# Row maxima of the attention scores taken in two parts instead of one

## What is computed

```python
def _attn_ref(q, k, v):
    q_pool = q.reshape(B, H, S // factor, factor, D).mean(axis=3)
    scores = scale * np.matmul(q_pool, k.transpose(0, 1, 3, 2))
    scores = scores - np.max(scores, axis=-1, keepdims=True)
    attn = np.exp(scores)
    attn = attn / (np.sum(attn, axis=-1, keepdims=True) + 1e-09)
    return np.matmul(attn, v)
...
x = attn_out.transpose(0, 2, 1, 3).reshape(B * S, H * D)
h = x @ w_in
g = np.maximum(h, 0.0) + alpha * np.minimum(h, 0.0)
return g @ w_out
```

## Time and profile before

| what | us |
|---|---|
| median of 3 runs | 893.23 (893.14 to 893.24) |
| profiled execution | 892.93 |
| its span, first to last instruction | 891.2 |
| TensorE busy in it | 859.3 |
| VectorE busy | 514.0 |
| ScalarE busy | 422.1 |

### The profile page before, as it was taken

One profiled execution on the slowest core, in us unless ns is written; L12 is line 12 of the kernel. 1 busy time (PEld: TensorE's weight loads), 2 busy tenths in 40 slices (PEclk: granted clock), 3 DMA queues, 4 the chain that ended last, 5 costly groups with the idle time before them and its releaser, 6 DMA issues. The chain is left out here.

```text
span 891.2 us, 19945 instructions
## 1 busy us (share of the span) xinstructions
PE 859.3 (96%) x6577; PEld 613.0 (69%) x6577; DVE 514.0 (58%) x791; ACT 422.1 (47%) x936; POOL 205.2 (23%) x170
## 2 busy tenths in 40 slices
PE   6899999999999999999999999999999999999996
PEld 3455555555555555555557999998999998999985
DVE  4676777677777777767674344345444445344342
ACT  2666666666666666666663222224222224222222
POOL 3101010110101010110402322323233233322320
PEclk9999999999999999999999999999999999999999
DMA  8626543464435543464122122124222223322211
GB/s 194 147 65 153 130 115 96 114 152 98 124 97 137 134 110 100 111 152 109 51 85 70 59 60 70 60 61 128 64 67 59 62 68 100 90 60 70 59 35 71
DMA packets 42638, 84.37 MB, mean 95 GB/s; under 512 B 7536, under 2 KB 15728, under 8 KB 42608
## 3 DMA queue, kind: packets, MB, share of 16 engines
q1 hardware_dynamic: 40208, 79.28, 34.6%
q10 hardware_dynamic: 2400, 4.72, 1.6%
HBM read 79.18 MB, written 4.79 MB: 94 GB/s over the span
## 5 line engine op out<-in xcount | busy, mean ns | idle before, releaser
L743 PE MATMUL slot_ps<-ff 128*128 128x384 f32 x1152 | 218.0, 337 | 1.4 <-PEq L740 1.4
L743 PEld LDWEIGHTS slot_ps<-ff 128*128 128x128 f32 x1152 | 204.4, 188 | 11.1 <-issue 3.2
L529 DVE TENSOR_REDUCE neg_max<-s_ps 128x1 f32<-128x1152 f32 x144 | 194.7, 1352 | 19.9 <-DVEq L528 19.1
L759 PE MATMUL s_ps<-ff 128*128 128x512 f32 x720 | 182.4, 394 | 2.6 <-PEq L756 2.6
L657 PE MATMUL s_ps<-k_f,q_f 64*128 64x512 f32 (+1 forms) x640 | 164.3, 632 | 1.0 <-PEq L709 0.9
L435 ACT ACTIVATE e_sb<-s_ps,neg_max 128x1024 f32<-128x1024 f32 x144 | 159.8, 1110 | 0.0
L690 PE MATMUL pv_ps<-pt,v_f 128*64 128x256 f32 (+1 forms) x1152 | 155.1, 412 | 0.2 <-PEq L709 0.2
L759 PEld LDWEIGHTS s_ps<-ff 128*128 128x128 f32 x720 | 133.4, 188 | 27.1 <-issue 4.1
L690 PEld LDWEIGHTS pv_ps<-pt,v_f 128*64 128x64 f32 x1152 | 76.7, 136 | 95.8 <-issue 52.6
L581 DVE TENSOR_SCALAR e_sb<-slot_ps,alpha_sb 128x384 f32<-128x384 f32 x96 | 59.3, 617 | 115.1 <-DVEq L579 115.1
L353 POOL TENSOR_TENSOR q_raw<-q_raw 128x576 f32<-128x576 f32 x30 | 42.2, 1406 | 343.8 <-POOLq L352 343.8
(11 more groups left out here) (42 smaller groups left out, 511.5 us busy)
## 6 DMA issues: line engine op xcount, KB each, us to landing
k_f<-in_k SPq DMA_DIRECT2D x64, 288.0 KB, 4.3
q_raw<-in_q SPq DMA_DIRECT2D x62, 288.0 KB, 4.2
wi_raw<-in_w_in SPq DMA_DIRECT2D x48, 256.0 KB, 2.6
wo_raw<-in_w_out SPq DMA_DIRECT2D x48, 256.0 KB, 2.6
v_f<-in_v SPq DMA_DIRECT2D x32, 288.0 KB, 3.8
out<-pt ACTq DMA_DIRECT2D x6, 768.0 KB, 4.8
inv_bc<-sums SPq DMA_DIRECT2D x32, 80.0 KB, 3.7
k_end<-in_k SPq DMA_DIRECT2D x64, 32.0 KB, 3.9
```

Of the source, the lines that this page charges most:

```text
L529: nc.vector.tensor_reduce(out=neg_max[:, b:b + 1], in_=s_ps[:, S_AT[b]:S_AT[b] + NKEY], op=ALU.max, axis=AX_X, negate=True).then_inc(max_r ...
L743: ins = nc.tensor.matmul(slot_ps[h][:, 0:TOK], w[i][:, d * P:(d + 1) * P], x[h][:, d * TOK:(d + 1) * TOK], start=(d == 0 and w is wi_hi an ...
L759: ins = nc.tensor.matmul(y_ps[h][t], g[h][:, t * P:(t + 1) * P], w[i], start=(first == 0 and j == 0), stop=(last == 1 and j == 2))
```

## The change

`row_max` stays for the first two tiles only. For all others the maximum is formed in parts. `big_max(s + 2)` reduces the 1024 columns of the large piece into `neg_big`. In even steps it is placed ahead of the wait for bank 2 and the ninth copy. Behind that copy, `small_max` reduces the small pieces of both tiles s+2 and s+3, two runs of 128 columns in bank 2, by one instruction into two columns of `neg_small`; `both_max` waits for the reductions and joins the two parts with a minimum (the maxima are negated) of one column. In odd steps there are `big_max` and `both_max` alone, since the small piece's maximum is there. The semaphore `even_cut_done`, its wait on VectorE and its increment on ScalarE go, since an odd step's reduction no longer touches bank 2.

```diff
             def exponential_cut(s, done=None):
...
-                                     accum_out=row_sum[:, 0, SUM_AT[t]:SUM_AT[t] + 1]).then_inc(done, 1)
+                if done is not None:
+                    ins.then_inc(done, 1)
...
-                    exponential_cut(s + 1, even_cut_done)
+                    exponential_cut(s + 1)
...
+            def big_max(s):
+                b = s % 2
+                dve.wait_ge(s_ready, 2).then_inc(s_ready, -2)
+                nc.vector.tensor_reduce(out=neg_big[:, b:b + 1],
+                                        in_=s_ps[:, S_AT[b] + BIG_AT[b]:S_AT[b] + BIG_AT[b] + 2 * BANK],
+                                        op=ALU.max, axis=AX_X, negate=True).then_inc(max_self, 1)
+
+            def small_max():
+                cols = s_ps[:, 2 * BANK:3 * BANK].rearrange("p (i c) -> p i c", c=P)[:, 0:4:3, :]
+                nc.vector.tensor_reduce(out=neg_small[:, :], in_=cols, op=ALU.max, axis=AX_X,
+                                        negate=True).then_inc(max_self, 1)
+
+            def both_max(s, parts):
+                b = s % 2
+                dve.wait_ge(max_self, parts).then_inc(max_self, -parts)
+                nc.vector.tensor_tensor(neg_max[:, b:b + 1], neg_big[:, b:b + 1], neg_small[:, b:b + 1],
+                                        ALU.min).then_inc(max_ready, 1)
...
+                if left > 1 and s % 2 == 0:
+                    big_max(s + 2)
                 if s % 2 == 0:
                     dve.wait_ge(bank2_ready, 1).then_inc(bank2_ready, -1)
                     nc.vector.tensor_copy(ninth_columns(ninth_tiles(s)),
                                           ninth_blocks(ninth_tiles(s))).then_inc(ninth_free, 1)
                 if left > 1:
-                    if s % 2 == 1:
-                        dve.wait_ge(even_cut_done, 1).then_inc(even_cut_done, -1)
-                    row_max(s + 2)
+                    if s % 2 == 0:
+                        small_max()
+                        both_max(s + 2, 2)
+                    else:
+                        big_max(s + 2)
+                        both_max(s + 2, 1)
```

More of the change, by code:

```diff
@@ L84, in build @@
         neg_max = sb("neg_max", [P, 2])
+        neg_big = sb("neg_big", [P, 2])
+        neg_small = sb("neg_small", [P, 2])
         table = sb("table", [P, 1])
@@ L153, in build @@
         s_ready = sem("s_ready")
+        max_self = sem("max_self")
         max_ready = sem("max_ready")
         exp_cut_done = sem("exp_cut_done")
-        even_cut_done = sem("even_cut_done")
         exp_done = sem("exp_done")
@@ L423, in _, with exponential_cut @@
         def _(act):
-            def exponential_cut(s, done):
+            def exponential_cut(s, done=None):
                 t, b, e = s % TILES, s % 2, s % 3 * NKEY
@@ L427, in exponential_cut @@
                 act.wait_ge(max_ready, 1).then_inc(max_ready, -1)
-                nc.scalar.activation(e_sb[:, e + END[b][0]:e + END[b][0] + P], s_ps[:, at:at + P],
-                                     ACT.Exp, bias=neg_max[:, b:b + 1],
-                                     accum_out=row_sum[:, 0, SUM_AT[t]:SUM_AT[t] + 1]).then_inc(done, 1)
+                ins = nc.scalar.activation(e_sb[:, e + END[b][0]:e + END[b][0] + P], s_ps[:, at:at + P],
+                                           ACT.Exp, bias=neg_max[:, b:b + 1],
+                                           accum_out=row_sum[:, 0, SUM_AT[t]:SUM_AT[t] + 1])
+                if done is not None:
+                    ins.then_inc(done, 1)
             def exponential(s):
```

## The result

| kernel | median us (runs) | ratio to before, 95% interval |
|---|---|---|
| before | 893.13 (20) | |
| changed | 894.96 (20), 894.05 to 895.78 | 1.0021 (1.0014 to 1.0028) |

The changed kernel is 1.8 us slower: a loss of 0.2%, and outside the range 887.3 to 894.0. Its runs spread over 1.7 us, those of before over 0.65. Its profiled execution took 894.15 (span 892.4), 0.8 under its median.

The account below looks back on a forecast made before the run. TensorE, busy for 96% of the span, was taken as the bound, so only its waits could shrink: 0.9 + 0.2 + 0.6 + 0.7 = 2.4 us off the profiled 892.93 gives 890.5, median 890.8; range 887.3 to 894.0.

Parts of the forecast that it names:

- the price of the join: VectorE's minimum of both parts: 0.15 waiting plus 0.15 work, 0.30 us behind the reduction; bounds 0.15 and 0.50.
- a join over 0.40: Sign to look for in the profile after: such a join would make the forecast wrong towards slower.
- the walk: Start times followed through one attention cycle of 18 steps (two head pairs), with the new order and prices.
- Step 2: Cycle's third step: ninth-block transposes start at 196.20 rather than 195.76, 0.44 us lost, made up two steps later.
- step 6: Ninth-block transposes behind step 5's inversion: TensorE still waits about 0.9 us, starting at 208.20 against 208.32.
- The cycle: 18 attention steps of two head pairs: gains 0.03 us in steps 0 to 7, 0.08 and 0.09 at two later steps.
- The opening: First attention steps, 2 to 6, without products to hide waits: earlier maxima give 0.9 us, once.
- B: Rival, larger gain: no 0.15 gap ahead of a join, some 3 us more come through, 887.8 us; chance 0.15.
- C: Rival, no change: 0.24 idle ahead of the odd maximum is VectorE's restart behind the slot copy, 893.0 us; chance 0.25.
- D: Rival, slower: VectorE becomes the bound of steps 0 to 6, joins cost 0.50, 896.5 us; chance 0.15.
- step 10: In each cycle, the odd maximum behind step 9's inversion comes 0.08 us sooner: 8 x 0.08 = 0.6 us.
- steps 0 and 14: Even steps with scaling and inversion ahead of the ninth copy: the large piece makes the even maximum 0.5 us later.

Follow-up runs that it names:

- one-input kernel: The changed kernel with the join done as a reduction over two columns of one tile instead of a two-input operation: 890.64 us, ratio 0.9972.
- the old form with the two-input join: The changed kernel with one whole reduction and the old wait again in pairs of steps whose even step inverts: 895.27 us, ratio 1.0031.
- the pair of idle operations: The kernel before with an unused VectorE operation behind each row maximum but the first two, with two inputs or one: 894.5 and 892.75 us.

## Why the prediction was wrong, point by point

**The step that failed is the price of the join**, "0.15 of work", "0.15" from below and "0.50" from above. It was taken from the inversion's sum as the nearest row in kind. That sum also has two inputs in SBUF, but in the trace of before it met GpSimd only once, for the last 0.05 us of a subtraction (446.67), and took 0.152 to 0.156 in all 32 places, so its rows could not show that price. In the one-input kernel it met one for longer and took 0.398: the row was nearest in kind, down to the price that it hid. In the changed kernel the join costs 0.159 in 112 places and up to 2.25 in 30, and this is worth 894.96 - 890.64 = 4.3 us. The upper bound of 0.50 came from a restart that turned out not to exist, and the mean of the joins lies well under it: 0.27, or 0.42 with the gap. The prediction's own sign, a join over 0.40, appeared in 24 places. The mean was not the point; the walk looked at three engines and not at GpSimd, which was busy for 23% of the span and off the path.

The trace of before had the clue, outside attention. GpSimd's own subtractions in the network, by source line (shortest, median, longest), and the longest of them in the timeline with VectorE beside it:

```profile
L394 POOL TENSOR_TENSOR ff<-wo_raw,ff x48: 1271/1294/2363, 476.2 to 870.5; 128x512 fp32r<-128x512 f32 x48
```

```profile
607.92 1.76 DVE L622 TENSOR_TENSOR ff<-x_f,ff 128x1536 fp32r<-128x1536 f32 x1 [0.82 <-DVEq L621]
...
608.47 2.36 POOL L394 TENSOR_TENSOR ff<-wo_raw,ff 128x512 fp32r<-128x512 f32 x1 [3.98 <-POOLq L393]
```

VectorE ends at 609.68, and GpSimd's 2.36 end 1.15 later, a little less than its usual length of 1.29: there it was GpSimd that waited for a two-input instruction of VectorE. All four such instructions of VectorE in that trace find a subtraction of GpSimd, which takes 2.35 or 2.36. A longest of 2.36 beside a median of 1.29 is what should have led me there.

The Trainium skill, page "SBUF — State Buffer", section "Who interferes with whom", says that a VectorE instruction with two SBUF inputs contends with a GpSimd instruction that reads SBUF, since its second input comes through the shared read interface, that the order of issue decides who blocks, and that `tensor_reduce` never contends on trn2. The traces agree: joins that end 0.02 behind GpSimd's addition, the reverse at 608.47, and 0.155 to 0.157 for the reducing join. By that page's rule the two-input join was the wrong choice, and the prediction did not weigh it.

**What was right.** All from the kernel with the one-input join, unless said:
- The prices of the pieces, and 0.15 ahead of each join (21.7 us before 142 joins in that kernel).
- Step 2 loses 0.44: measured 0.43 in each cycle but the first (0.53). Step 4 makes it up, step 6 waits 0.84 (about 0.9 was said), and each start came within 0.05 of the walk. The ninth transposes of step 2 show no wait in brackets, though; the wait stands ahead of the big scores before them (0.28).
- The cycle: forecast 0.20 (0.03 + 0.08 + 0.09), measured 0.18 to 0.22 in each of five, and 0.46 in the first, which stays open. The opening: 0.9 forecast, 0.78 measured.
- The sum: 890.8 forecast, 890.64 measured. That it fits within 0.2 is in part luck. At its last instruction TensorE is 2.26 ahead of before: 0.78 from the opening and 1.48 from the next six cycles, less 0.21 by which it starts later and 0.19 from 418 us to the end of attention, and 0.4 more from the network (1.87 ahead at 600 us, 2.23 at 700), which the forecast had at nothing.
- In the changed kernel itself only the opening's gain came through, 0.77 at 70 us, although three joins had been long by then.

**The rivals.** B (no gap ahead of a join) is out: the gap is in all 142 places. C (a restart behind the slot copy) is out: after the change the odd large piece starts where the copy ends, at 193.20 behind 192.59 + 0.69, with no idle time.

```profile
192.59 0.69 DVE L587 COPY pt<-slot_ps 128x512 f32<-128x512 f32 x1
...
193.20 1.22 DVE L540 TENSOR_REDUCE neg_big<-s_ps 128x1 f32<-128x1024 f32 x1
```

D (VectorE as the bound) named the side on which it ended, and put the deciding point 0.1 above the join's 0.30. The mean excess, 16.0 / 142 = 0.11, lies at just that point. But its mechanism, a join of 0.50 everywhere, is not what happened: one in five was hit, by up to 2.1 us, and what it costs depends on whether TensorE needs that tile at that time. With the same order and a join of 0.155 the time is 890.64, so VectorE is not the bound that D meant. D's own terms, 890.8 + 5.6 + 0.6 for step 10, come to 897.0 and not to 896.5.

**What was left on the table.** The prediction priced the reordering at step 2 as a loss of 0.44 that is made up two steps later. It is made up only because waits there shrink anyway (0.54 from step 2 to step 4, with or without the loss): with the loss taken out, all of it comes through, 3.1 us. That was not a wrong number, but an order that the walk had already named as late ("that is steps 0 and 14") and that the experiments show to be worth undoing.

## What to carry to other kernels

Before a small VectorE operation with two SBUF inputs goes on a critical chain, look at what GpSimd does beside it, however idle that engine is, and at the longest and not only the mean duration of like rows; a reduction over two columns of one tile, or a per-partition scalar as second operand, cost the same or 0.06 more and was never held up. Splitting a reduction pays where the engine otherwise idles for the second part's input (even steps without an inversion ahead), and here hardly anywhere else: the best kernel, 885.8, has the split in just the steps in which the copy waits, plus the odd ones outside inversions. A cost that comes from a collision moves with the phase of the two engines, so an edit that saves time elsewhere can make it larger; remove the collision before measuring the edit.

## What the runs showed of the hardware

- A VectorE operation with two inputs in SBUF that starts while GpSimd runs an addition or subtraction ends 0.01 to 0.02 us after that instruction: 128x1 took 0.91, 0.97, 1.41 and 2.25 us instead of 0.16. The inversion's sum did the same (0.398 instead of 0.156). A join that begins ahead of GpSimd's instruction (40.32 against 40.41) or together with it (443.94) takes 0.16; one that began 0.01 behind took 1.41.
- An operation of VectorE in the network with one input in PSUM and one in SBUF started beside GpSimd's work in 7 places of the changed kernel, and its 96 durations lie between 0.556 and 0.559: not held.
- GpSimd's one-input scaling of 0.67 us holds a join up as well (0.36 us); VectorE's one-input joins (0.155 to 0.157) and those with a per-partition scalar (0.212 to 0.217) were not held up once in 142 places each, some 30 of which began while GpSimd was working.
- The reverse holds: a subtraction of 1.29 us on GpSimd took 2.36 behind one of 1.76 on VectorE.
- Whether such collisions make a kernel vary more from run to run is not shown. Between the fastest and the slowest run lie 1.7 us (changed kernel), 6.6 (the old form with the two-input join, where the two longest runs had a granted clock of 0.996 and the others 0.998 or more) and 0.2 (one-input join); but the pair of idle operations has 1.0 with 29 long ones and 1.1 with none.
